# Scores from one pass of 128 rows and remainder products of 64 rows, in a fused attention and two-expert-stage kernel

## What is computed

```python
batch, n_heads, seq, head_dim = (2, 8, 1152, 64)

def _attn_ref(q, k, v):
    B, H, S, D = q.shape
    factor = 2
    scale = 1.0 / np.sqrt(D)
    q_pool = q.reshape(B, H, S // factor, factor, D).mean(axis=3)
    scores = scale * np.matmul(q_pool, k.transpose(0, 1, 3, 2))
    scores = scores - np.max(scores, axis=-1, keepdims=True)
    attn = np.exp(scores)
    attn = attn / (np.sum(attn, axis=-1, keepdims=True) + 1e-09)
    return np.matmul(attn, v).astype(np.float32)

def reference(**kwargs):
    attn_out = _attn_ref(**attn_kwargs)
    x = np.ascontiguousarray(attn_out.transpose(0, 2, 1, 3)).reshape(B * S, H * D)
    x = _moe_ref(x=x, **moe_kwargs)
    return _moe2_ref(x=x, **moe2_kwargs)
```

## Time and profile before

| | us |
|---|---|
| median of 3 runs (lowest to highest) | 897.13 (896.65 to 897.86) |
| profiled execution, its own time | 895.97 |
| its span, first to last instruction | 894.3 |
| TensorE busy in the span | 839.8 (94%) |
| VectorE, ScalarE, GpSimd busy | 398.5, 315.7, 208.4 |
| mean granted TensorE clock | 0.968 |
| products on the `QTh` line, 240, and the `QTl` line, 240 | 87.4 and 81.4 |
| mean recorded time of one 512-column product (line 466) | 0.395 |

### The profile page before, as it was taken

The page is one execution under the profiler, slowest core; times in us unless marked ns, Lnnn a source line. Parts: engine busy times, 40 slices in busy tenths (PEclk is TensorE's granted clock), DMA queues, the critical chain, the costliest instruction groups (busy, mean ns, idle before and its releaser), DMA issues.

```text
span 894.3 us, 13134 instructions
## 1 busy us (share of the span) xinstructions
PE 839.8 (94%) x4716; PEld 717.2 (80%) x4717; DVE 398.5 (45%) x646; ACT 315.7 (35%) x514; POOL 208.4 (23%) x179
## 2 busy tenths in 40 slices
PE   7999999999979999999999999999997089999996
PEld 7787778787858998898989998898986068878885
DVE  3775857676763413321414213321413312696235
ACT  3555656564642412220303112220315012675233
POOL 5845865595321000000000000000000501232012
PEclk9999999999989999999999999999998579999998
DMA  8834334342442202110112002110000531596410
GB/s 203 273 85 121 79 86 114 94 106 67 122 131 95 95 1 95 32 64 1 34 61 94 0 0 94 38 58 1 1 1 0 190 140 47 178 330 235 146 42 19
DMA packets 30105, 79.83 MB, mean 89 GB/s; under 512 B 4007, under 2 KB 4007, under 8 KB 30064
## 3 DMA queue, kind: packets, MB, share of 16 engines
q1 hardware_dynamic: 26944, 69.99, 25.7%
q0 software_dynamic: 2960, 8.68, 3.0%
q10 hardware_dynamic: 160, 0.59, 0.3%
HBM read 69.52 MB, written 10.78 MB: 90 GB/s over the span
## 4 chain that ended last, share of the span: by engine, by line
PE 86%; DMA 3%; DVE 3%; POOL 2%; issue 2%; ACT 2%; SPq 0%; POOLq 0%; DVEq 0%; ACTq 0%
PE L L409 23%; PE L L466 23%; PE ring L385 8%; PE scores L350 8%; PE L L581 8%; PE L L555 7%; PE ring L364 5%; PE scores L373 1%; DMA xr<-sorted_rows 1%; DVE negmax L787 1%; POOL sorted_rows L1132 1%; ACT a L612 1%; PE L L563 1%; DMA rawQ<-in_qT 1%; DMA out<-o,destc 1%
## 5 line engine op out<-in xcount | busy, mean ns | idle before, releaser
L409 PE MATMUL L<-xTh,w1h 128*128 128x384 f32 x384 | 129.7, 338 | 6.1 <-DVE w1l L750 6.1
L409 PE MATMUL L<-xTh,w1l 128*128 128x384 f32 x384 | 129.5, 337 | 0.0
L409 PE MATMUL L<-xTl,w1h 128*128 128x384 f32 x384 | 129.4, 337 | 0.0
L658 ACT ACTIVATE hh<-L 128x384 fp32r<-128x384 f32 x96 | 46.6, 491 | 201.3 <-PE L L409 201.3
L466 PE MATMUL L<-w2h,hh 128*128 128x512 f32 x288 | 114.3, 397 | 0.0
L466 PE MATMUL L<-w2h,hl 128*128 128x512 f32 x288 | 113.8, 395 | 0.0
L466 PE MATMUL L<-w2l,hh 128*128 128x512 f32 x288 | 113.7, 395 | 0.0
L886 DVE SCALAR_TENSOR_TENSOR hl<-L,hh 128x384 fp32r<-128x384 f32 x96 | 52.9, 557 | 123.7 <-ACT hh L658 123.3
L1132 POOL DMA_INDIRECT sorted_rows<-acc,posi x9 | 10.7, 1186 | 414.3 <-DVE posi L976 411.9
L612 ACT ACTIVATE a<-scores,negmax 128x1152 f32<-128x1152 f32 x72 | 87.9, 1221 | 37.2 <-DVE negmax L787 37.2
L787 DVE TENSOR_REDUCE negmax<-scores 128x1 f32<-128x1152 f32 x72 | 97.2, 1350 | 3.2 <-PE scores L350 3.0
(11 more groups left out here) (169 smaller groups left out, 1355.8 us busy)
## 6 DMA issues: line engine op xcount, KB each, us to landing
raw<-in_v SPq DMA_DIRECT2D x48, 512.0 KB, 6.0
raw<-in_w SPq DMA_DIRECT2D x32, 512.0 KB, 5.2
rawK<-in_kT SPq DMA_DIRECT2D x32, 288.0 KB, 4.7
rawQ<-in_qT SPq DMA_DIRECT2D x30, 288.0 KB, 5.9
sorted_rows<-filler SPq DMA_DIRECT2D x19, 257.0 KB, 6.0
V<-in_vr SPq DMA_DIRECT2D x16, 288.0 KB, 3.1
xr<-sorted_rows POOLq DMA_DIRECT2D x15, 257.0 KB, 3.0
rawQ<-in_qT ACTq DMA_DIRECT2D x2, 288.0 KB, 6.5
```

Of the source, the lines that this page charges most:

```text
L409: last = pe.matmul(L1[i % L1_BANKS][:, 0:CW], w[:, d, wf], x[:, cols], start=(n == 0), stop=(n == 3 * DT - 1))
L658: act.activation(hh[c % 2][:, f, :], L1[i % L1_BANKS][:, 0:CW], ACT.Relu) \
```

## The change

`KT` now holds the high part of K in both halves, a new buffer `KTl` the low part in both, and `Qhl` (in place of `QTl`) the high part of Q in the upper half and the low part in the lower. One product of 128 rows, `Qhl` times `KT`, gives high x high + low x high. The remaining high x low is a product of 64 rows, taken from the upper half (`Qhl`, `KTl`) for chunks 0 and 2 and from the lower half (`QTh`, `KTl`) for chunk 1. The product low x low is no longer made. The order of a tile is: the full products of all chunks, then chunk 0 in the upper and chunk 1 in the lower half (alternating over the heads), then chunk 2. The semaphore `s_ready` is set by the last. Preparation makes one more copy (`Qhl`, upper half, with its semaphore `q_top`), subtracts K on 128 partitions instead of 64, and Q on 64 instead of 128; some waits are added.

```diff
-        QTl = [sb(f"QTl{i}", [P, AW], F32R, att) for i in range(2)]
+        Qhl = [sb(f"Qhl{i}", [P, AW], F32R, att) for i in range(2)]
         a = [sb(f"a{i}", [P, SEQ], F32, att) for i in range(3)]
+        KTl = [sb(f"KTl{i}", [P, SEQ], F32R, att) for i in range(2)]
...
                     pe.wait_ge(S["k_lo"], 2 * j + (k == XT) + 1)
+                    pe.wait_ge(S["q_top"], 2 * j + (k == XT) + 1)
                     pe.wait_ge(S["q_lo"], 2 * j + (k == XT) + 1)
...
+                top, low = slice(0, DH), slice(DH, P)
+
+                def product(c, Q, K, s, cols, rows_, **kw):
+                    return pe.matmul(scores[g % 2][:, c, 0:SW], Q[s][rows_, cols], K[s][rows_, c * SW:(c + 1) * SW], **kw)
+
                 for c in chunks:
-                    keys = slice(c * SW, (c + 1) * SW)
-                    n = 0
-                    for s, cols in heads:
-                        for Q in (QTh, QTl):
-                            last = pe.matmul(scores[g % 2][:, c, 0:SW], Q[s][:, cols], KT[s][:, keys],
-                                             start=(n == 0), stop=(n == 2 * len(heads) - 1))
-                            n += 1
-                    if c == SC - 1:
-                        last.then_inc(S["s_ready"], 1)
+                    for n, (s, cols) in enumerate(heads):
+                        product(c, Qhl, KT, s, cols, slice(0, P), start=(n == 0), stop=False)
+                for n, (s, cols) in enumerate(heads):
+                    product(0, Qhl, KTl, s, cols, top, start=False, stop=(n == len(heads) - 1))
+                    product(1, QTh, KTl, s, cols, low, start=False, stop=(n == len(heads) - 1))
+                for n, (s, cols) in enumerate(heads):
+                    last = product(2, Qhl, KTl, s, cols, top, start=False, stop=(n == len(heads) - 1))
+                last.then_inc(S["s_ready"], 1)
...
             copy(QTh[0][:, 0:QS], qs[:], scale=SCALE).then_inc(S["q_hi"], 1)
+            copy(Qhl[0][0:DH, 0:QS], qs[0:DH, :], scale=SCALE).then_inc(S["q_top"], 1)
...
                 pool.wait_ge(S[f"kq_in{s}"], 64 * (p + 1))
+                pool.wait_ge(S["q_lo"], n)
                 pool.tensor_copy(KT[s][:], rawK[s][:]).then_inc(S["k_hi"], 1)
                 pool.wait_ge(S["k_hi"], n + 1)
-                pool.tensor_tensor(KT[s][DH:P, :], rawK[s][DH:P, :], KT[s][DH:P, :].bitcast(F32),
-                                   ALU.subtract).then_inc(S["k_lo"], 1)
+                pool.tensor_tensor(KTl[s][:], rawK[s][:], KT[s][:].bitcast(F32), ALU.subtract).then_inc(S["k_lo"], 1)
...
                 pool.tensor_copy(QTh[s][:, cols], qs[:]).then_inc(S["q_hi"], 1)
+                pool.tensor_copy(Qhl[s][0:DH, cols], qs[0:DH, :]).then_inc(S["q_top"], 1)
                 pool.wait_ge(S["q_hi"], n + 1)
-                pool.tensor_tensor(QTl[s][:, cols], qs[:], QTh[s][:, cols].bitcast(F32), ALU.subtract) \
+                pool.wait_ge(S["q_top"], n + 1)
+                pool.tensor_tensor(Qhl[s][DH:P, cols], qs[DH:P, :], QTh[s][DH:P, cols].bitcast(F32), ALU.subtract) \
                     .then_inc(S["q_lo"], 1)
...
             for j in range(PAIRS):
+                pool.wait_ge(S["q_lo"], 2 * j + 2)
                 if j:
                     spread_pair(j - 1)
```

More of the change, by code:

```diff
@@ L252, in spread_blocks @@
             return N_STEP[k] if j and k in N_STEP else ()
-        names = """consts_in kq_in0 kq_in1 v_in0 v_in1 k_hi k_lo q_sum q_scaled q_hi q_lo s_ready max_ready
+        names = """consts_in kq_in0 kq_in1 v_in0 v_in1 k_hi k_lo q_sum q_scaled q_hi q_top q_lo s_ready max_ready
             exp_ready den_ready rinv_ready t_ready0 t_ready1 t_ready2 nb_ready a_out0 a_out1 a_out2 o_ready o_low o_high spread_ready y_ready pads_ready emb_in
@@ L844, in _ @@
             dve.wait_ge(S["k_hi"], 1)
-            tt_(KT[0][DH:P, :], rawK[0][DH:P, :], KT[0][DH:P, :].bitcast(F32), ALU.subtract) \
+            tt_(KTl[0][:], rawK[0][:], KT[0][:].bitcast(F32), ALU.subtract) \
                 .then_inc(S["k_lo"], 1)
             dve.wait_ge(S["q_hi"], 1)
-            dve.scalar_tensor_tensor(out=QTl[0][:, 0:QS], in0=qs[:], scalar=SCALE, in1=QTh[0][:, 0:QS].bitcast(F32),
+            dve.scalar_tensor_tensor(out=Qhl[0][DH:P, 0:QS], in0=qs[DH:P, :], scalar=SCALE,
+                                     in1=QTh[0][DH:P, 0:QS].bitcast(F32),
                                      op0=ALU.mult, op1=ALU.subtract).then_inc(S["q_lo"], 1)
@@ L1058, in prep_k @@
                 pool.wait_ge(S[f"kq_in{s}"], 64 * (p + 1))
+                pool.wait_ge(S["q_lo"], n)
                 pool.tensor_copy(KT[s][:], rawK[s][:]).then_inc(S["k_hi"], 1)
                 pool.wait_ge(S["k_hi"], n + 1)
-                pool.tensor_tensor(KT[s][DH:P, :], rawK[s][DH:P, :], KT[s][DH:P, :].bitcast(F32),
-                                   ALU.subtract).then_inc(S["k_lo"], 1)
+                pool.tensor_tensor(KTl[s][:], rawK[s][:], KT[s][:].bitcast(F32), ALU.subtract).then_inc(S["k_lo"], 1)
             def prep_q(n, s):
                 cols = slice(0, QS) if s == 0 else slice(XW, AW)
+                pool.wait_ge(S["q_top"], n)
                 pool.wait_ge(S["q_lo"], n)
@@ L1092, in split_x @@
                     .then_inc(S["x_lo"], 1)
-            for Q in (QTh, QTl):
+            for Q in (QTh, Qhl):
                 pool.memset(Q[0][:, QS:AW].bitcast(F32), 0.0).then_inc(S["pads_ready"], 1)
@@ L1118, in _ @@
                 if j:
+                    pool.wait_ge(S["q_lo"], min(2 * j + 3, NH))
                     split_x(j - 1)
```

## The result

The changed kernel takes 899.61 us (median of 10 runs, 898.54 to 900.34); the kernel before, on the same chips, 896.69 (10 runs, 895.78 to 897.86). The ratio is 1.0033, with a 95% interval of 1.0023 to 1.0042: **slower by 2.9 us**. The profiled execution has a span of 898.7 us against 894.3.

The account below looks back on a forecast made before the run. The prediction took TensorE to bound the attention stage during `times_v`, with VectorE nearly the bound between. 2.8 us (stretches) plus 0.8 (start) gave +3.6 on a median of 897.13: 900.7 us, range 897.0 to 913.0.

Parts of the forecast that it names:

- No instruction goes away; halves pair up: Score products on TensorE: six per tile stay, neighbours in different halves run together, saving 0.174 us per tile, 0.35 with two heads.
- 0.27 of drain and 0.10 of load on entry: TensorE entering half-row products: 0.27 us from last full product's start to the load, plus 0.10 load, 0.37 for the pair.
- 0.02 later for the scores, 0.17 for the transposes: Ordinary one-head tile: scores complete 0.02 us later and the transposes start 0.17 us later than before.
- +0.20 and +0.19 per stretch: Stretches between two `times_v`: next `times_v` 0.20 us later, or 0.19 with the two-head tile; 14 stretches by 0.20, +2.8 us.
- The shared tile ends earlier but brings nothing: Tile of two heads: scores complete 0.15 to 0.16 us earlier, transposes unchanged; the loop can't use the earlier scores.
- Start +0.8: First stretch: GpSimd's added copy for head 1 is uncovered, 0.75 us; +0.8 us for that stretch as a whole.
- Sum: Whole kernel: 2.8 for the stretches plus 0.8 for the start, +3.6 us, forecast 900.7 us.
- the clock that rose earlier after the wait for expert weights: After the attention stage: where TensorE's clock rises again may move by a us or so, inside the range.
- (a): Rival on the half-row products, chance 0.15: the halves do not run together; 912 to 913 us.
- (b): Rival, chance 0.14: 64 rows of the same width need no drain, the pair saves 0.174 us per tile; 891.3 us.
- (c): Rival, chance 0.11: the drain costs the 0.27 us wait but not the load; 897.9 us.
- (d): Rival counted with the forecast, together 0.60: a pair's loads go one after the other; 0.04 to 0.1 more per tile, 902 to 904.

Follow-up runs that it names:

- the last experiment: Kernel before, with the shared tile's low x high products of two heads stacked into one of 128 rows: 893.34 us (5 runs), ratio 0.9956.

## Why the prediction was right

- **No instruction goes away; halves pair up.** Right. Each tile still makes six products, and the pair saves 0.18, shown by the run that has no pair.
- **0.27 of drain and 0.10 of load on entry.** Right to the hundredth, and from one 8-row product. Whether a half of 64 rows behaves like a strip of 8 was the weakest step of the argument; the run with a switch at each chunk shows both shares in both directions.
- **0.02 later for the scores, 0.17 for the transposes.** From the start of the first full product to that of the transposes it is 135.62 - 134.36 = 1.26; the transposes' record is 0.06 longer than in rows 3, so 1.32 until they begin in truth, where before it is 1.13 (132.65 to 133.78). That is +0.19; the 0.02 too much is within the rounding of the records.
- **+0.20 and +0.19 per stretch.** Measured 0.20 and 0.19, and the steps in between are the ones named. In the first kind the single transposes come 0.19, 0.03 and 0.19 later after the `times_v` before them, so the wait of 0.32 did swallow the second tile's delay; in the second kind it is 0.01, -0.03, 0.17 and 0.18, and the jump stands where the normalisation waits for the late spread transposes.
- **The shared tile ends earlier but brings nothing.** Right for the change (its drains undo it); the last experiment shows what that tile is worth when it ends earlier without them, 0.5 us per pair.
- **Start +0.8.** Too large: 0.58 until the first `times_v`. The copy cost 0.68 on GpSimd, not 0.75, and 0.67 at the shared tile, and 0.1 of that went in the stretch's slack. It is the term that was most mis-sized, by 0.2. That it is this copy is shown by the run with ScalarE's copy, and by the full-row run, whose first `times_v` is as late (35.46) without any half rows.
- **Sum.** 3.6 forecast, 3.25 in the trace up to the fifteenth `times_v`, 2.9 between the medians. Of the 0.7 too much, 0.2 is the start, 0.1 the rounding of 0.19 to 0.20, and 0.4 the clock that rose earlier after the wait for expert weights, which the forecast had named as able to move the time but not counted. The forecast of 900.7 rests on a median of 3 runs of before, 897.13, that lies 0.4 above that of ten.
- **The rivals.** (a) is excluded by the pair. Its price, 912 to 913, came out at 913.16, but partly by luck: against before, the 14 stretches brought 13.2 us and the start 3.6, with the clock low for longer there than in the changed kernel, where the forecast had 14 and about 2. (b) is excluded by the drain; the run with five products, which has the saving without the drain, takes 891.60, where (b) was given 891.3. (c) fell with the starts 0.37 apart. (d) did not show: the two loads of a pair start within 0.01 us.

The Trainium skill, TensorEngine Tiling (Array Packing), Key Properties, says that a change of the tiling mode drains TensorE; the traces agree, with 0.27 us from the last product's start to the next load in both directions. The Overview of the same page of the Trainium skill gives a factor of up to 2 for a contraction of at most 64; here it holds for the two neighbours themselves, which take one product time of 0.174, and is more than lost where three half products stand between two changes of mode.

## What to carry to other kernels

Half-row products have to stand in runs long enough to pay for the two changes of rows. Here (384 columns) a change there and back costs 0.37 + 0.33 us against 2 x 0.174 for going on, 0.35 more; a pair saves 0.174, so one pair between the changes loses, and two break even, as in the shared tile. That three would win is an estimate from these numbers; no run has them. Before counting saved products, ask in which tiles TensorE is what the others wait for: here two per stretch, so the ten products saved in a pair of heads brought the time of five. Two half-filled products of different heads that are added up anyway can be stacked into one of full rows, which saves the product without any change of mode.

## What the runs showed of the hardware

A change in the rows of a product costs the same as a change in its columns: the next load starts 0.26 to 0.27 us after the start of the last 384-column product (135.35 and 135.61; with columns 157.37 and 157.63). A load that comes after it adds 0.10, and is recorded within the product's duration (0.44 instead of 0.34). The loads of the upper and the lower half run side by side (135.06 and 135.07), which I had put at 0.04 to 0.1 apart as a possibility. On GpSimd a cast of 64x576 takes as long as one of 128x576 (0.66 and 0.67), and a subtraction on 128x1152 as long as one on 64x1152, as this row of the changed kernel beside rows 8 shows:

```profile
15.16 2.63 POOL L1070 TENSOR_TENSOR KTl<-rawK,KT 128x1152 fp32r<-128x1152 f32 x1
```
